# Windowed attention ahead of a two-layer and a mixture-of-experts MLP: attention in half tiles of 64 queries on the partition halves, 208 score columns, a negated mask taken with the minimum, and the output normalised instead of the probabilities

## What is computed

```python
B, H, S, D = 2, 8, 768, 64            # n_sink = 4, window = 128
scores = q @ k.T / sqrt(D)
keep = (pos_k < n_sink) | ((pos_q - pos_k >= 0) & (pos_q - pos_k < window))
scores = where(keep, scores, -1e9);  scores -= scores.max(-1)
a = exp(scores);  a = a / (a.sum(-1) + 1e-9);  out = a @ v
x = out as [B*S, H*D]                 # 1536 x 512
x = relu(x @ w_in)**2 @ w_out         # 512 -> 2048 -> 512
out = top-2 of 8 experts (512 -> 1024 -> 512), chosen by noisy logits
```

## Time and profile before

| | us |
|---|---|
| median of 3 runs (lowest, highest) | 842.13 (839.35, 842.53) |
| span of the profiled execution | 837.7 |
| PE busy | 759.9 (91%) |
| DVE busy | 377.1 (45%) |
| ACT busy | 312.7 (37%) |
| POOL busy | 103.7 (12%) |

### The profile page before, as it was taken

The page is one execution under the profiler, slowest core; times in us unless marked ns, Lnnn a source line. Parts: engine busy times, 40 slices in busy tenths (PEclk is TensorE's granted clock), DMA queues, the critical chain, the costliest instruction groups (busy, mean ns, idle before and its releaser), DMA issues.

```text
span 837.7 us, 14386 instructions
## 1 busy us (share of the span) xinstructions
PE 759.9 (91%) x3868; PEld 602.8 (72%) x3869; DVE 377.1 (45%) x967; ACT 312.7 (37%) x603; POOL 103.7 (12%) x85
## 2 busy tenths in 40 slices
PE   3659998999999999999980999999999999999993
PEld 1436665788788887888860888888888888888872
DVE  5988894452221532225555264426244254444120
ACT  2438996342222322233440343325243343343220
POOL 3650000000000030000304001101101101101101
PEclk9759999999999999999995899999999999999996
DMA  7913332200000020005205627253262717362211
GB/s 247 340 54 92 126 94 95 110 1 1 0 1 1 1 103 0 0 0 212 91 14 219 230 45 239 46 184 98 59 230 43 245 39 238 71 218 48 40 25 26
DMA packets 36587, 82.21 MB, mean 98 GB/s; under 512 B 6352, under 2 KB 6352, under 8 KB 36560
## 3 DMA queue, kind: packets, MB, share of 16 engines
q1 hardware_dynamic: 19264, 38.47, 14.0%
q10 hardware_dynamic: 11200, 29.36, 9.7%
q0 software_dynamic: 6096, 14.04, 8.5%
HBM read 62.27 MB, written 19.60 MB: 98 GB/s over the span
## 4 chain that ended last, share of the span: by engine, by line
PE 85%; DVE 5%; issue 4%; ACT 2%; SPq 1%; DMA 1%; DVEq 0%; POOL 0%; ACTq 0%; POOLq 0%
PE ps L1391 20%; PE ps L1356 19%; PE ps L1288 16%; PE ps L1278 15%; PE ps L1399 3%; PE ps L1177 3%; PE ps L1163 3%; PE ps L1201 2%; DVE s_probs L777 2%; PE ps L1346 2%; PE ps L1305 1%; DVE s_probs L745 1%; SPq L382 1%; PE ps L1299 1%; ACT s_probs L517 1%
## 5 line engine op out<-in xcount | busy, mean ns | idle before, releaser
L886 DVE SCALAR_TENSOR_TENSOR g_sb<-ps,g_sb 128x512 f32<-128x512 f32 x48 | 33.2, 692 | 124.1 <-ACT g_sb L569 123.0
L1125 DVE TENSOR_TENSOR hT_lo<-ps,hT_hi 128x1024 fp32r<-128x1024 f32 x29 | 35.5, 1225 | 115.2 <-ACT hT_hi L666 115.2
L484 POOL DMA_INDIRECT out<-y_sb,y_tok x29 | 45.1, 1554 | 330.7 <-ACT y_sb L655 330.7
L569 ACT ACTIVATE g_sb<-ps 128x512 f32<-128x512 f32 x48 | 28.7, 598 | 144.2 <-PE ps L1278 144.2
L655 ACT ACTIVATE y_sb<-ps,meta 128x512 f32<-128x512 f32 x29 | 19.9, 688 | 153.6 <-PE ps L1391 153.6
L1288 PE MATMUL ps<-w_hi,gT_hi 128*128 128x512 f32 x192 | 76.5, 399 | 0.4 <-DVE gT_lo L888 0.3
L1145 DVE TENSOR_TENSOR w_lo<-w_raw,w_hi x28 | 62.9, 2289 | 30.1 <-ACT w_hi L687 30.1
L1288 PE MATMUL ps<-w_lo,gT_hi 128*128 128x512 f32 x192 | 75.9, 395 | 0.0
L1288 PE MATMUL ps<-w_hi,gT_lo 128*128 128x512 f32 x192 | 75.7, 394 | 0.0
L468 POOL DMA_INDIRECT expert_rows<-x_rows,slots_i x24 | 26.1, 1087 | 372.5 <-DVE slots_i L992 366.1
L1391 PE MATMUL ps<-w_hi,hT_hi 128*128 x232 | 62.6, 413 | 2.7 <-DVE hT_lo L1125 2.7
(11 more groups left out here) (186 smaller groups left out, 1278.7 us busy)
## 6 DMA issues: line engine op xcount, KB each, us to landing
w_raw<-w ACTq DMA_DIRECT2D x28, 1024.0 KB, 9.0
xg<-expert_rows SPq DMA_DIRECT2D x30, 262.0 KB, 2.7
k_sb<-kT_near SPq DMA_DIRECT2D x8, 704.0 KB, 4.9
w_raw<-w_in SPq DMA_DIRECT2D x4, 1024.0 KB, 7.6
w_raw<-w_out SPq DMA_DIRECT2D x4, 1024.0 KB, 12.6
w_raw<-w SPq DMA_DIRECT2D x4, 1024.0 KB, 8.1
out<-pad_rows SPq DMA_DIRECT2D x13, 256.0 KB, 9.2
q_sb<-qT SPq DMA_DIRECT2D x8, 384.0 KB, 3.7
```

The lines of the kernel that those rows point to most:

```text
L484: pool.indirect_dma_start(out=out, out_offset=bass.IndirectOffsetOnAxis(ap=y_tok[:, :], axis=0), in_=y_sb[:, :], in_offset=None, compute_o ...
L569: act.activation(g_sb[:, b, :], ps[:, 4 + b, :], ACT.Relu).then_inc(m_relu, 1)
L886: dve.scalar_tensor_tensor(g_sb[:, b, :], ps[:, 4 + b, :], 0.0, g_sb[:, b, :], ALU.max, ALU.mult).then_inc(m_sq, 1)
L1125: dve.tensor_tensor(hT_lo[:, :, :].rearrange("p c s -> p (c s)"), ps[:, 2:4, :].rearrange("p a b -> p (a b)"), hT_hi[:, :, :].rearrange("p ...
```

## The change

Work goes in 24 batches (`BATCHES`), three per pair, of two query tiles. Each tile of 128 queries is two halves of 64 (`HQ`). The lower half's scores lie on PSUM partitions 0 to 63 and the upper half's on 64 to 127, so each half has a window of its own of 192 keys, and with 16 sinks a row has 208 columns (`COLS`). A score matmul covers 64 rows (a head) and 64 columns (a half) of the array; a batch has 16 of them, eight with 192 and eight with 16 columns, all in one group with one signal at its end.

The mask is positive: the scores out of PSUM are multiplied by minus the scale, the mask is added, and the row minimum is the exponential's bias, with scale -1. ACT's exponentials stay unnormalised. PE transposes columns 0 to 127 and 128 to 207 of each of a batch's four units (two tiles, two heads); ACT copies the first ones and DVE the others. PV now has the probabilities as weights and v as the moving operand: 16 matmuls of 64 columns, and the output has queries on partitions. DVE multiplies it by the inverse sum (`s_norm`), and PE turns it by two transposes (`s_turn`). v is stored once for every offset of 64 (`runs`) and once as tails of 64 keys and 16 sinks (`tails`), so that each half finds its keys from partition 0.

SP loads q, k, v and v_tail of a pair together, once both scores and outputs of the pair two before are done; the zeros for out come after attention and after the second half of the MLP weights. `short_ready` is signalled before the masks are built. The loops over turns are written out.

```diff
-SINKS = 32
-SHORT_COLS = 2 * P + SINKS
-LOADS = 5
-AHEAD = 3
+SINKS = 16
+HQ = P // 2
+WIN = P + HQ
+COLS = WIN + SINKS
+TAIL = COLS - P
+LOADS = 4
+PB = QT // 2
+BATCHES = PAIRS * PB
...
             def load_pair(pair, slot):
                 sp.dma_start(q_sb[:, slot, :], qT[:, pair, :]).then_inc(qkv_in[slot], 16)
-                sp.dma_start(k_sb[:, slot, :], kT_near[:, pair, :]).then_inc(qkv_in[slot], 16)
-                sp.dma_start(v_sb[:, slot, :], v[:, pair, :]).then_inc(qkv_in[slot], 16)
-                load_sinks(pair, slot)
+                sp.dma_start(k_sb[:, slot, :], kT[:, pair, :]).then_inc(qkv_in[slot], 16)
+                sp.dma_start(v_sb[:, slot, :, :, :].rearrange("p t h d -> p (t h d)"), v[:, pair, :]).then_inc(qkv_in[slot], 16)
+                sp.dma_start(vt_sb[0:TAIL, slot, :, :, :].rearrange("p t h d -> p (t h d)"), v_tail[:, pair, :])\
+                  .then_inc(qkv_in[slot], 16)
...
+            with sp.If(short == 1):
+                for pair in range(2, PAIRS):
+                    sp.wait_ge(s_scores, PB * (pair - 1))
+                    sp.wait_ge(s_pv, PB * (pair - 1))
+                    load_pair(pair, pair % 2)
...
+            sp.wait_ge(attn_done, 1)
+            for i in range(4):
+                sp.dma_start(piece(w_raw, 1, i), mlp_source(1, i)).then_inc(w_piece[i], 16)
             sp.wait_ge(consts_done, 1)
             for t in range(CAP // P):
                 sp.dma_start(out[t * P:(t + 1) * P, :], pad_rows[:, 0:DM]).then_inc(out_zeroed, 16)
...
+            def s_soften(n):                                # ACT
+                buf = n % BUFS
+                for u in range(4):
+                    a = s_probs[:, buf, u, :]
+                    act.wait_ge(s_masked, 4 * n + u + 1)
+                    act.activation(a, a, ACT.Exp, bias=s_min[:, buf, u:u + 1], scale=-1.0,
+                                   accum_out=s_sum[:, buf, u:u + 1]).then_inc(s_exp, 1)
...
+                for n in range(BATCHES):                    # ACT
+                    if n + 2 < BATCHES:
+                        s_soften(n + 2)
+                    if n + 1 < BATCHES:
+                        s_copy_main(n + 1)
+                    if n >= 1:
+                        s_high(n - 1)
...
+            def s_mask(n):                                  # DVE
...
+                for u in range(4):
+                    st, hh = u // 2, u % 2
+                    qt = n % PB * 2 + st
+                    dve.tensor_tensor_reduce(s_probs[:, buf, u, :], ps[:, 2 * (n % 2) + hh, st * COLS:(st + 1) * COLS],
+                                             bias[:, min(qt, 2), :], -SCALE, 3.0e38, ALU.add, ALU.min,
+                                             s_min[:, buf, u:u + 1]).then_inc(s_masked, 1)
+            def s_copy_tail(n):
+                dve.wait_ge(s_T, n + 1)
+                dve.tensor_copy(s_probsT[0:TAIL, n % 2, 1::2, :], four(REST, TAIL)).then_inc(s_T_tail, 1)
...
+            def s_norm(n):
+                dve.wait_ge(s_inverted, n + 1)
+                dve.wait_ge(s_pv, n + 1)
+                dve.tensor_tensor(o_sb[:, n % 2, :, :], ps[:, PV, 0:2 * P].rearrange("p (u d) -> p u d", u=4),
+                                  s_inv[:, n % BUFS, :].unsqueeze(2).to_broadcast([P, 4, DH]), ALU.mult).then_inc(s_normed, 1)
...
+                for n in range(BATCHES):                    # DVE
+                    if n + 2 < BATCHES:
+                        s_mask(n + 2)
+                    if n + 1 < BATCHES:
+                        s_copy_tail(n + 1)
+                        s_invert(n + 1)
+                    s_norm(n)
+                    if n >= 1:
+                        s_low(n - 1)
...
+            def s_score(n):                                 # PE
+                slot = n // PB % 2
+                if n % PB == 0:
+                    pe.wait_ge(qkv_in[slot], 16 * LOADS * (n // PB // 2 + 1))
...
+                for st in range(2):
+                    for at, size, k_at in ((0, WIN, None), (WIN, SINKS, P + SEQ)):
+                        for hh in range(2):
+                            a = slice(hh * DH, (hh + 1) * DH)
+                            for h in range(2):
+                                t = 2 * (n % PB * 2 + st) + h
+                                k0 = t * HQ if k_at is None else k_at
+                                m = pe.matmul(ps[h * HQ:(h + 1) * HQ, 2 * (n % 2) + hh, st * COLS + at:st * COLS + at + size],
+                                              q_sb[a, slot, t * HQ:(t + 1) * HQ], k_sb[a, slot, k0:k0 + size], start=True, stop=True)
+                m.then_inc(s_scores, 1)
+            def s_transpose(n):
...
+                for u in range(4):
+                    pe.wait_ge(s_exp, 4 * n + u + 1)
+                    pe.transpose(four(MAIN, P)[:, u, :], s_probs[:, buf, u, 0:P], ident[:, :])
+                    t = pe.transpose(four(REST, TAIL)[:, u, :], s_probs[:, buf, u, P:COLS], ident[:, :])
+            def s_output(n):
...
+                for u in range(4):
+                    st, hh = u // 2, u % 2
+                    for chunk, (rows, v_t) in enumerate(((P, v_sb), (TAIL, vt_sb))):
+                        for h in range(2):
+                            t = 2 * (n % PB * 2 + st) + h
+                            m = pe.matmul(ps[h * HQ:(h + 1) * HQ, PV, u * DH:(u + 1) * DH],
+                                          s_probsT[0:rows, n % 2, 2 * u + chunk, h * HQ:(h + 1) * HQ], v_t[0:rows, slot, t, hh, :],
+                                          start=(chunk == 0), stop=(chunk == 1))
...
+                for n in range(BATCHES):                    # PE
+                    if n + 2 < BATCHES:
+                        s_score(n + 2)
+                    if n + 1 < BATCHES:
+                        s_transpose(n + 1)
+                    s_output(n)
+                    if n >= 1:
+                        s_turn(n - 1)
+                s_turn(BATCHES - 1)
```

More of the change, by code:

```diff
@@ new lines, in build @@
+        pt_at = short_mem.at
+        s_probsT = short_mem.place("s_probsT", [P, 2, 8, P], F32)
+        s_min, s_sum, s_inv = (short_mem.place("s_" + n, [P, BUFS, 4], F32) for n in ["min", "sum", "inv"])
+        first_mem = Memory(nc, pt_at, short_mem.at)
+        rel_t = first_mem.place("rel_t", [P, 2, COLS], F32)
+        key_t = first_mem.place("key_t", [P, 3, COLS], F32)
+        near = first_mem.place("near", [P, 2, COLS], BF16)
+        sink = first_mem.place("sink", [P, 3, COLS], BF16)
@@ L274, in carry, with batch_out, four @@
             eng.sem_inc(carried[eng], 1)
[L276 to L295, removed]
+        def batch_out(t, n):
+            c, at = n // PB % DC, n // PB // DC * SEQ + n % PB * 2 * P
+            return t[:, c, at:at + 2 * P]
+        MAIN, REST, PV, TURNED = 4, 5, 6, 7
+        def four(bank, rows):
+            return ps[0:rows, bank, :].rearrange("p (u s) -> p u s", u=4)
         def value_of_routed(eng):
@@ L800, in s_turn @@
-            def s_turn(i, last):
-                for j in range(TURN):
-                    s_step(i, j, last, True)
-            dve.sem_inc(x_lo_done, 1)
+            dve.sem_inc(short_ready, 1)
+            dve.wait_ge(near_done, 2)
+            then(dve.tensor_scalar(near[:, :, :], rel_t[:, :, :], window_f, MASKED, ALU.is_ge, ALU.mult))
+            then(dve.tensor_scalar(sink[:, :, :], key_t[:, :, :], n_sink_f, MASKED, ALU.is_ge, ALU.mult))
+            then(dve.tensor_tensor(bias[:, 0, :], sink[:, 0, :], near[:, 0, :], ALU.max))
@@ L1154, in _ @@
         def _(pe):
-            def s_score(i, j):
-                slot, qt = j // QT, j % QT
-                n, sinks = near_keys(qt)
-                at, size = (2 * P + (qt - 2) * SHORT_COLS, SHORT_COLS) if sinks else (0, n)
-                for hh in range(2):
-                    a = slice(hh * DH, (hh + 1) * DH)
-                    m = pe.matmul(ps[:, 2 * (j % 2) + hh, 0:size], q_sb[a, slot, qt * P:(qt + 1) * P],
-                                  k_sb[a, slot, at:at + size], start=True, stop=True)
-                    m.then_inc(s_scores, 1)
@@ L1220, in _, with s_turn @@
+            def s_turn(n):
+                pe.wait_ge(s_normed, n + 1)
+                if n >= 1:
+                    pe.wait_ge(x_lo_done, n)
+                for st in range(2):
+                    t = pe.transpose(ps[:, TURNED, st * P:(st + 1) * P],
+                                     o_sb[:, n % 2, 2 * st:2 * st + 2, :].rearrange("p u d -> p (u d)"), ident[:, :])
+                t.then_inc(s_oT, 1)
             pe.wait_ge(short_ready, 1)
```

365 lines of the change are left out of this document (126 added, 239 removed).

## The result

The changed kernel takes 852.97 us (median of four runs, 851.62 to 856.9); the kernel before, run beside it, 841.64 (839.35 to 842.53). The ratio is 1.0152, 95% interval 1.0117 to 1.0187: 1.5% slower. The profiled executions have spans of 849.2 and 837.7, 11.5 apart. The last subtract of attention ends at 148.3 instead of 139.3, so 9.0 of the 11.5 lie in attention.

What follows compares the result with a forecast made beforehand. TensorE paced the kernel before; each pair's loads would pace it after. Pair 2 at 36.5, 17.0 us per pair, S(21) at 122.0, attention's end 140.4 against 139.3: 1.1 us more, 843.2 us, range 829 to 860.

Steps and rivals of the forecast that it cites:

- The likeliest case: Whole kernel: late pair loads take what the split and shorter steps give back; 843.2 us, own range 836 to 851, chance 0.50.
- S, T, O and U: TensorE's scores, transposes, PV and output turning per batch: 1.01, 1.03, 1.05, 0.37 us; S(n) is batch n's scores.
- Rival A: TensorE's scores: array quarters run only two at a time, 1.88 us per batch; +16 us, 859; chance 0.12.
- rival E: DVE-ACT ring with a stopped copy, late mask, bubbles in the unrolled instruction stream: +6 us, 849; chance 0.05.
- Rival D: Pair loads bind nowhere, so attention's steps run at 3.5 us: about 806; chance 0.03.
- The size of the load: Loads of q, k, v and v_tail per pair: 8.0 us plus 0.3 for release and wake, 8.3.
- Pair 2: First pair load behind the MLP weights: weights land about 26.5, release 28.2, pair 2 lands at 36.5 us.
- The clock: TensorE after each load gap: 4.8 us at 1.2 GHz, costing 2.1 us, between 0 and 3.
- rival B: TensorE's clock does not come back in the 8.7 us between two gaps: +20 us, 863; chance 0.12.
- rival C: Gaps ahead of scores are mild, shorter loads and clock up at once or never down: -16 us, 827; chance 0.18.
- The split: POOL's weight split beside attention: only the add is exposed, costing 0.5 us against 17 before; 3 if the copy stops.
- The start: Attention's beginning: first scores at 10.7 us, bound by data, low clock until about 21, third batch's PV done at 28.2.

Runs made afterwards that it cites:

- before, split held back: The kernel before, with GpSimd's split of the first half of w_in and w_out held back until attention has ended: 846.07 us.
- order of need, no addition, one by one: As order of need, no addition, but the four w_in and w_out loads go singly behind pairs 2, 3, 4 and 5: 804.44 us.
- order of need, no addition: As order of need, with DVE's addition of 1e-9 left out and the reciprocal taken of the sum directly: 803.65 us.
- order of need: As two waits, with pair 2's load ahead of w_in and w_out, these in twos behind pairs 2 and 3, router's loads behind the last pair: 812.26 us.
- two waits: Changed kernel, q and k asked for after the scores two pairs earlier, v and v_tail after their PV, with separate waits on TensorE: 818.05 us.
- the run that kept it up: Changed kernel with 22 unused 128-column matmuls on TensorE ahead of the first scores of pairs 4 to 7: 845.61 us.

## Why the prediction came out as it did

Forecast 843.2 within 829 to 860; measured 852.97. The likeliest case was the right one in its mechanism, and its number was 9.8 too low, outside its own 836 to 851: it called no change what is 1.5% slower. Attention's end in seven kernels, one profiled execution of each, gives the account. Each row is compared with the one above it; what stands behind the difference is what the two kernels differ in:

```
before                                          139.3
before, split held back                         122.0   -17.3  the split
order of need, no addition, one by one          101.8   -20.2  steps 3.48 for 4.12, S(0) at 7.9 for 11.8
order of need, no addition                      103.3    +1.5  w_raw in twos
order of need                                   109.9    +6.6  the addition, held by the split
two waits                                       118.0    +8.1  w_raw and the router's loads ahead of pair 2
the change                                      148.3   +30.3  one release and one wait for all four loads
```

- TensorE's work. For S, T, O and U 1.01, 1.03, 1.05 and 0.37 were predicted, and 1.00, 1.03, 1.08 and 0.37 measured. Rival A, quarters two at a time (859), is refuted by S. The step of 3.48 is the sum of these four, so rival E's ring and bubbles don't show in it. The Trainium skill (TensorEngine Tiling (Array Packing), Tiling Modes) lists 64x64 as four independent tiles; here the trace agrees, with 32 instructions in 1.00 us.
- The joint wait was the right mechanism, shown by the run with two waits: the same work and bytes, 35 us less. Rival D, loads that bind nowhere, was wrong for this kernel. Its price of 806, with some 8 us for POOL in it, compares with the order of need and the addition in place, 812.26: about right, and 6 too low.
- The size of the load, the first term that failed. From q's issue to S I took 8.3 us; measured were 11.5 for pair 2 and 8.9, 8.8, 9.3, 10.0 and 9.2 for the five behind it, 4.7 more in these five. The rest of their periods came out 0.7 shorter than I had it. The periods were 17.49, 17.22, 17.59, 19.53 and 17.62 where I had 17.5 and then 17.0 four times: +4.0. My rate of 402 GB/s came from a stretch with other loads; leaving out v_tail's 0.49 MB took 1.9 us from a load, which is 0.49 MB / 1.9 = 258 GB/s at its end. (My lower bound for the load, 7.3, took a fixed part of 1.7 us where the row beside it gives 2.0; with that it is 7.5.) In pair 5 SyncE spent 1.82 us on the issue of k, where it spent 0.43 in the others. Why the loads took 3.3 us more in all without the addition, and up to 10.6 with the router's loads moved, I can't explain.
- Pair 2, the second. The release came at 28.08, as predicted (28.2), but the data came at 39.6, not at 36.5: +3.1. I had w_raw land at 26.5, at 400 GB/s; it landed at 33.3, and pair 2 behind it. In this window the DMA engines were busy 0.98 of the time, and moved 318 GB/s:
```profile
4.50:30.00 25.50, 16.57 (x331) 14.16 (x331) 15.29 (x71) 13.14 (x48) 6.31 (x19) 1.00 0.98 318
```
 I suspected the router's loads, which hold SyncE for 7.84 and 3.69 us; moved away, they bring S(6) only 0.8 forward. That the rate is the rest is argued, not shown.
- The end: +0.9, since from S(21) to attention's end it took 19.3 us instead of 18.4. 3.1 + 4.0 + 0.9 = 8.0, attention's end at 148.3 for 140.4. Behind it the first MLP matmul starts 2.7 us after the last subtract (150.98) where I had 2.1 as before: 0.6. The low clock then lasts until 156.2, 5.2 us into the MLP, where it lasted 3.6 before (141.4 to 145.0): by my estimate 0.8 more. That makes 9.4 of the 9.8.
- The clock. 2.1 us per gap were predicted, and 1.85 measured by the run that kept it up. I had 4.8 us of work at the low level behind a gap; from S(3p) to the rise it was 4.0, 3.5, 3.4, 6.3, 3.8 and 3.3. It came back between any two gaps, so rival B is refuted. The gap ahead of S(9) was mild, 1.45, but it doesn't price a mild gap: the clock was already low when it began. It had fallen behind the wait of 2.37 us for o_sb, which I had not counted as a cost in clock. The other five gaps were 5.08 to 7.76, so rival C, mild gaps at 827, is out too.
- The split. 0.5 us was predicted, and in the changed kernel's time nothing can be measured of it: its largest hold, 3.87, made TensorE wait 2.37, and without the addition the kernel was not faster. The load of pair 3 covered that wait; it was not harmless. Once the gaps are gone the same addition costs 8.6 us. In the kernel before, the split cost attention 17.3, as I had read from the missing stages.
- The start. S(0) came at 12.6, not 10.7, on v_tail of pair 0 (the last of the four loads); with q and k alone it starts at 7.9. That the release still came as predicted is luck, two errors that cancel. I had the low clock last until about 21; it ended at 16.2, so that S(2) and O(0) took 1.0 and 1.1 us, not 1.8 and 1.9.

## What to carry to other kernels

A faster inner step is worth only what its inputs' lead allows. Read how far ahead of its use each load is asked for, from the release to the consumer, and split a release and a wait by who needs the data: here one for all four loads turned a gain of 21 us in attention (139.3 to 118.0) into a loss of 9. Order the queue by need: bulk loads that are wanted only at attention's end belong behind the next pair's. An operation held by another engine can look free while another wait covers it; price it with that wait gone.

## What the hardware did that I had not expected

- POOL's split on SBUF holds DVE's addition of a 128x4 tile to 3.87 us, but not the reciprocal of the same tile at 0.16, also from SBUF to SBUF, nor a copy of 80x512 out of PSUM at 0.68. The trace of the kernel before shows it within one subtract of POOL, where the reciprocal takes 0.15 and a like small multiply right behind it 4.39, until that subtract ends:
```profile
36.86 4.50 POOL L456 TENSOR_TENSOR w_lo<-w_raw,w_hi 128x2048 fp32r<-128x2048 f32 x1
36.92 0.15 DVE L769 RECIPROCAL s_inv<-s_inv 128x2 f32<-128x2 f32 x1
36.99 4.39 DVE L753 TENSOR_SCALAR s_neg<-s_max 128x2 f32<-128x2 f32 x1
```
 The Trainium skill (VectorE: DVE Perf Modes, What auto-detection actually checks) says that an operation can take the mode with both read ports if a single source and the destination are in SBUF and their outermost dimensions are even or equal. The addition has that form and was held; the copy, out of PSUM, hasn't and wasn't. The reciprocal has it too and wasn't held; the section says that a built-in operation is capped by what firmware enables, and doesn't name the reciprocal.
- Two loads of 16 KB for the router took 7.84 and 3.69 us of SyncE's time right behind the first pairs in the changed kernel, 2.60 and 2.63 in the same place of the kernel before, and 1.83 and 2.84 behind the last pair (the version of 803.65). No run shows what makes the difference.
- Loads of the same bytes, with nothing else on the queue, took from 8.5 to 10.6 us from q's issue to S in one kernel (the router's last, pairs 3 to 6). I had one duration for all.
